# Attention and two feed-forward layers on one core: six spaced batches of transposes a job, a second bank for narrow tiles, layer two's weights kept on chip

## The reference

```python
# q, k, v: (4, 8, 576, 64); token blocks of 64; a row sees its own and earlier blocks
scores = scale * np.matmul(q, k.transpose(0, 1, 3, 2))
scores = np.where(mask, scores, -1000000000.0)
attn = exp(scores - max);  attn = attn / (sum(attn) + 1e-09)
x = (attn @ v) laid out as (2304 tokens, 512)
h = x @ w_in;   x = (h * sigmoid(h)) @ w_out            # d_ff = 2048
h = x @ w_in2;  y = (h * sigmoid(1.702 * h)) @ w_out2
```

## Time and profile before

| | |
|---|---|
| median of 3 runs | 1049.69 us (1048.61 to 1050.72) |
| profiled execution | 1050.25 us, span 1048.5 us |
| PE busy | 991.5 us, 95% |
| DVE, ACT, POOL busy | 44%, 33%, 13% |
| mean granted PE clock | 0.982 |

### The profile page before, as it was taken

The page is one execution under the profiler, slowest core; times in us unless marked ns, Lnnn a source line. Parts: engine busy times, 40 slices in busy tenths (PEclk is TensorE's granted clock), DMA queues, the critical chain, the costliest instruction groups (busy, mean ns, idle before and its releaser), DMA issues.

```text
span 1048.5 us, 13460 instructions
## 1 busy us (share of the span) xinstructions
PE 991.5 (95%) x5256; PEld 778.6 (74%) x5256; DVE 464.5 (44%) x861; ACT 346.4 (33%) x751; POOL 141.3 (13%) x118
## 2 busy tenths in 40 slices
...
GB/s 291 226 252 200 223 231 192 214 202 215 190 213 202 216 192 214 198 213 193 181 185 236 200 198 229 419 198 198 175 231 200 193 201 208 200 185 218 198 312 30
DMA packets 41614, 222.12 MB, mean 212 GB/s; under 512 B 4560, under 2 KB 6096, under 8 KB 19024
## 3 DMA queue, kind: packets, MB, share of 16 engines
...
...
## 4 chain that ended last, share of the span: by engine, by line
PE 78%; DVE 12%; ACT 6%; issue 2%; DMA 2%; POOL 0%; SPq 0%; DVEq 0%; POOLq 0%
PE ps_h L550 12%; PE ps_h L552 12%; PE ps_h L551 12%; PE ps_y L566 11%; PE ps_y L569 10%; PE ps_y L568 10%; PE ps_a L530 4%; DVE p_sb L770 4%; PE ps_a L519 3%; DVE g_f L794 2%; PE ps_a L498 2%; ACT p_sb L637 2%; ACT sig L659 2%; DVE q_lo L752 2%; DMA k_raw<-kT 1%
## 5 line engine op out<-in xcount | busy, mean ns | idle before, releaser
L794 DVE SCALAR_TENSOR_TENSOR g_f<-sig,ps_h 128x512 f32<-128x512 f32 (+1 forms) x160 | 101.3, 633 | 361.1 <-ACT sig L659 361.1
L659 ACT ACTIVATE sig<-ps_h 128x512 f32<-128x512 f32 (+1 forms) x160 | 88.8, 555 | 399.5 <-PE ps_h L552 399.5
L550 PE MATMUL ps_h<-x_hi,w_hl 128*128 128x512 f32 (+1 forms) x444 | 176.3, 397 | 0.3 <-DVE x_lo L746 0.2
L566 PE MATMUL ps_y<-g_hi,w_hl 128*128 128x512 f32 (+1 forms) x444 | 174.6, 393 | 0.5 <-DVE g_lo L800 0.5
L552 PE MATMUL ps_h<-x_lo,w_hl 128*128 128x512 f32 (+1 forms) x444 | 165.8, 373 | 0.0
L569 PE MATMUL ps_y<-g_lo,w_hl 128*128 128x512 f32 (+1 forms) x444 | 165.6, 373 | 0.0
L551 PE MATMUL ps_h<-x_hi,w_hl 128*128 128x512 f32 (+1 forms) x444 | 165.3, 372 | 0.0
L568 PE MATMUL ps_y<-g_hi,w_hl 128*128 128x512 f32 (+1 forms) x444 | 164.7, 371 | 0.0
L800 DVE SCALAR_TENSOR_TENSOR g_lo<-g_f,g_hi 128x512 fp32r<-128x512 f32 (+1 forms) x160 | 105.9, 662 | 72.2 <-ACT g_hi L667 72.2
L667 ACT ACTIVATE g_hi<-g_f 128x512 fp32r<-128x512 f32 (+1 forms) x160 | 94.2, 589 | 109.2 <-DVE g_f L794 108.9
L519 PE MATMUL ps_a<-ident,p_sb 128*128 128x128 f32 x384 | 67.8, 287 | 41.1 <-DVE pt_sb L775 26.4
...
## 6 DMA issues: line engine op xcount, KB each, us to landing
...
```

What stands on the lines that cost most here:

```text
L550: nc.tensor.matmul(dst, lo, x_hi[t % 2][:, k, 0:w], start=(k == 0), stop=False)
L566: nc.tensor.matmul(dst, lo, g_hi[:, c % 2, 0:w], start=(f == 0 and (t > 0 or k % 2 == 0)), stop=False, skip_group_check=True)
L659: nc.scalar.activation(sig[:, 0:w], ps_h[:, 0:w], ACT.Tanh, scale=0.5 * ALPHA[c // SECOND]).then_inc(s_sig, 1)
L794: nc.vector.scalar_tensor_tensor(g_f[:, 0:w], sig[:, 0:w], 1.0, ps_h[:, 0:w], ALU.add, ALU.mult).then_inc(s_g, 1)
```

## The change

1. **Batches.** Eight batches of transposes a job become six of four 128x128 transposes each: the two single ones (row 0's last block, row 7) ride with a batch of three. They are further apart (`BATCH_AT`). ACT and DVE take three batches each; a mixed batch is taken in two copies.
2. **Lanes.** In early jobs the batches alternate between `ps_a`'s bank 2 and `ps_y`'s bank 3, and a batch waits for the take of the batch before the last one. The score rows that had used `ps_y` go back to `ps_a`, so early units wait for the exps of the rows before them (`UNIT_FREE`).
3. **Normalizing.** Row 7 is a group of its own. The places of every DVE and ACT step (`MAX_AFTER` ... `SPLIT_AFTER`) are now tables, for early and later jobs; `queries_low` moves from 14 to 8 places before its job, `keys_low` from 18 to 7 in POOL's order, `keys_high` from 18 to 16.
4. **Two banks.** In 256-token tiles `hidden(c)` alternates between `ps_h` and a spare bank, `g_f` is halved, tanh is written into it in place of `sig`; PE then waits for the gate of chunk `c - 2`. In 512-token tiles one bank remains.
5. **Weights.** `RING` is 6. Layer two's 16 split chunks are loaded once into memory that the attention and layer one used (`w_all`), no longer once a tile.

```diff
-GROUPS = ((0, 1), (1, 3), (3, 5), (5, 8))
+GROUPS = ((0, 1), (1, 3), (3, 5), (5, 7), (7, 8))
...
-BATCHES = [((0,), 0, 4), ((0,), 4, 5), ((1,), 0, 4), ((2,), 0, 4), ((3,), 0, 3), ((4,), 0, 3), ((5, 6), 0, 2), ((7,), 0, 1)]
+BATCHES = ((((0,), 0, 4),), (((1,), 0, 4),), (((2,), 0, 4),), (((3,), 0, 3), ((0,), 4, 5)), (((5, 6), 0, 2),),
+           (((4,), 0, 3), ((7,), 0, 1)))
 NBATCH = len(BATCHES)
-NORMED = (1, 1, 2, 3, 4, 5, 7, 8)
-ON_ACT = {0: 1, 3: 2, 5: 3, 6: 4}
-ON_DVE = {1: 1, 2: 2, 4: 3, 7: 4}
+NORMED = (1, 2, 3, 4, 7, 8)
+ON_ACT = {0: 1, 2: 2, 4: 3}
+ON_DVE = {1: 1, 3: 2, 5: 3}
+N_ON = 3
...
-RING = 4
-MORE = 7
-RING2 = RING + MORE
+RING = 6
+ATT_SLOTS = 8
+STAGE_SLOT = ATT_SLOTS
+RAW_SLOT = ATT_SLOTS + 1
+RING_SLOT = ATT_SLOTS + 2
+SLOT_BYTES = 2 * CW * 4
...
-START = [28 * n - STEP for n in range(FIRST)] + [8 * 13 + 32 * n for n in range(JOBS - FIRST)]
-UNIT_AT = ((0, 5, 10, 15, 20), (0, 6, 12, 18, 24))
-BATCH_AT = ((9, 11, 14, 16, 19, 21, 27, 29), (8, 10, 14, 16, 20, 22, 30, 32))
-PV_AT = (31, 34)
-
-UNIT_FREE = ((0, 0, 1, 3, 5), (0, 1, 3, 5, 7))
+START_AT = (-8, 20, 48, 77, 106)
+START = list(START_AT) + [START_AT[FIRST] + 2 * NF * n for n in range(1, JOBS - FIRST)]
+UNIT_AT = ((0, 5, 9, 13, 21), (0, 6, 14, 18, 26))
+BATCH_AT = ((12, 14, 21, 24, 26, 31), (6, 15, 18, 22, 26, 30))
+PV_AT = (34, 32)
+
+MAX_AFTER = (0, 2)
+EXP_AFTER = ((1, 1), (3, 3))
+INVERT_AFTER = (3, 3)
+MULTIPLY_AFTER = ((6, 6), (4, 5))
+TAKE_AFTER = (-1, 1)
+SPLIT_AFTER = ((1, 2), (1, 2))
+
+PREP_AT = (16, 15, 8, 7)
+
+UNIT_FREE = (0, 1, 3, 5, 7)
...
-PREP = {START[n] - 18: n for n in range(1, JOBS)}
+MAXIMA = {p + MAX_AFTER[late(n)]: (n, u) for p, (n, u) in UNIT.items()}
+EXPS = [{p + EXP_AFTER[late(n)][i]: (n, UNITS[u][i]) for p, (n, u) in UNIT.items() if i < len(UNITS[u])} for i in range(2)]
+INVERT = {p + INVERT_AFTER[late(n)]: (n, u) for p, (n, u) in UNIT.items()}
+MULTIPLY = [{p + MULTIPLY_AFTER[late(n)][i]: (n, u, UNITS[u][i]) for p, (n, u) in UNIT.items() if i < len(UNITS[u])}
+            for i in range(2)]
+TAKE = {p + TAKE_AFTER[late(n)]: (n, b) for p, (n, b) in BATCH.items()}
+SPLIT = [{p + SPLIT_AFTER[late(n)][i]: n for p, n in VALUE.items()} for i in range(2)]
+PREP = [{START[n] - p: n for n in range(1, JOBS)} for p in PREP_AT]
...
+def other(c):
+
+    return c % 2 if TILES[c // NF][1] < TMAX else 0
+
+
+def second_slot(j):
+
+    return j if j < RING_SLOT else RING_SLOT + (j - RING_SLOT + SECOND - RING) % RING
+
+
+def gates_before(c):
+
+    return c - 1 if c and other(c) != other(c - 1) else c
...
-        def row_bank(n, r):
-
-            if n < FIRST and r in (1, 2, 5, 6):
-                return ps_y[:, 512 * (3 - r % 2):512 * (4 - r % 2)]
+        def lane(n, b):
+
+            return ps_y[:, 1536:2048] if n < FIRST and b % 2 else bank(2)
+
+        def row_bank(r):
             return bank(0 if r in (0, 7) else 1 - r % 2)
...
+            if c < SECOND:
+                return w_hl[:, c % RING, low, col:col + P]
+            return w_all[:, second_slot((c - SECOND) % NF), low, col:col + P]
+
+        def hidden_of(c):
+            w = TILES[c // NF][1]
+            spare = ps_y[:, 1024:1024 + w] if c < NF else ps_a[:, 0:w]
+            return spare if other(c) else ps_h[:, 0:w], g_f[:, w * other(c):w * other(c) + w]
...
+            def load_second(j):
+
+                if j == 0:
                     sp.wait_ge(s_xl, NK * PER)
-                else:
-                    sp.wait_ge(s_y, c - RING2 + 1)
-                dst = w_hl[:, s, :, :] if s < RING else w_more[:, s - RING, :, :]
-                sp.dma_start(dst.rearrange("p a c -> p (a c)").bitcast(F32), w_split[i, :, :]).then_inc(s_ld[s], 16)
+                if j == STAGE_SLOT:
+                    sp.wait_ge(s_st, 16 * 2 * NF)
+                if j == RAW_SLOT:
+                    sp.wait_ge(s_w, 2 * NF)
+                if j >= RING_SLOT:
+                    sp.wait_ge(s_y, SECOND - RING + j - RING_SLOT + 1)
+                sp.wait_ge(s_st, 16 * (NF + j + 1))
+                sp.dma_start(w_all[:, second_slot(j), :, :].rearrange("p a c -> p (a c)").bitcast(F32),
+                             w_split[NF + j, :, :]).then_inc(s_l2[j], 16)
...
-                limit = c + 3 if c + 3 < SECOND + RING else c + RING2 - 1
-                while ahead <= min(limit, NCHUNK - 1):
-                    load_split(ahead)
-                    ahead += 1
+                if NF <= c + RING - 1 < SECOND:
+                    load_split(c + RING - 1)
+                if SECOND - NF <= c < SECOND - NF + RING_SLOT:
+                    load_second(c - SECOND + NF)
...
-                    if place in PREP:
-                        keys_low(PREP[place])
+                    if place in PREP[3]:
+                        keys_low(PREP[3][place])
...
-                if n or UNIT_FREE[0][u]:
-                    pe.wait_ge(s_ex, ROWS * n + UNIT_FREE[late(n)][u])
+                if n or u:
+                    pe.wait_ge(s_ex, ROWS * n + UNIT_FREE[u])
...
-                elif b - 1 in ON_ACT:
-                    pe.wait_ge(s_ta, 4 * n + ON_ACT[b - 1])
                 else:
-                    pe.wait_ge(s_td, 4 * n + ON_DVE[b - 1])
+                    before = b - 2 if n < FIRST else b - 1
+                    if before in ON_ACT:
+                        pe.wait_ge(s_ta, N_ON * n + ON_ACT[before])
+                    if before in ON_DVE:
+                        pe.wait_ge(s_td, N_ON * n + ON_DVE[before])
...
+                    if c == 0:
                         pe.wait_ge(s_exl, 2)
+                    elif gates_before(c):
+                        pe.wait_ge(s_g, gates_before(c))
...
+                h, g = hidden_of(c)
+                if gates_before(c):
+                    act.wait_ge(s_gl, gates_before(c))
                 act.wait_ge(s_h, c + 1)
-                nc.scalar.activation(sig[:, 0:w], ps_h[:, 0:w], ACT.Tanh,
-                                     scale=0.5 * ALPHA[c // SECOND]).then_inc(s_sig, 1)
+                nc.scalar.activation(g, h, ACT.Tanh, scale=0.5 * ALPHA[c // SECOND]).then_inc(s_sig, 1)
```

More of the change, by code:

```diff
@@ L166, in build @@
-        k_raw = sb(att, "k_raw", [P, 2, S])
-        q_end = sb(att, "q_end", [P, 2, 2, BLK])
-        q_hi = sb(att, "q_hi", [P, 2, SQ - 2 * BLK], F32R)
-        q_lo = sb(att, "q_lo", [P, 2, SQ - 2 * BLK], F32R)
-        k_hi = sb(att, "k_hi", [P, 2, S], F32R)
-        k_lo = sb(att, "k_lo", [P, 2, S], F32R)
-        v_sb = sb(att, "v_sb", [P, 2, NJ, P])
-        p_sb = sb(att, "p_sb", [P, PCOLS])
-        att.close()
-        w_more = sb(ctx, "w_more", [P, MORE, 2, CW], F32R)
+        first = ExitStack()
@@ new lines, in build @@
+        q_lo = sb(first, "q_lo", [P, 2, SQ - 2 * BLK], F32R)
+        k_hi = sb(first, "k_hi", [P, 2, S], F32R)
+        k_lo = sb(first, "k_lo", [P, 2, S], F32R)
+        v_sb = sb(first, "v_sb", [P, 2, NJ, P])
+        p_sb = sb(first, "p_sb", [P, PCOLS])
+        pt_sb = sb(first, "pt_sb", [P, 2, NJ, SQ])
+        used = 2 * P + 5 * BLK + 4 * ROWS + 2 * (SQ + S) + 4 * (SQ - 2 * BLK + S) + 2 * NJ * P + PCOLS + 2 * NJ * SQ
+        sb(first, "rest", [P, ATT_SLOTS * SLOT_BYTES // 4 - used])
+        stage = sb(first, "stage", [P, 2, CW], F32R)
@@ L223, in build @@
         s_st = sem("s_st")
-        s_ld = [sem(f"s_ld{i}") for i in range(RING2)]
+        s_ld = [sem(f"s_ld{i}") for i in range(RING)]
+        s_l2 = [sem(f"s_l2{i}") for i in range(NF)]
         s_xh = sem("s_xh")
@@ L279, in weights, with pieces @@
-        def weights(c, low, col):
-            s = slot_of(c)
-            ring, s = (w_hl, s) if s < RING else (w_more, s - RING)
-            return ring[:, s, low, col:col + P]
+        def pieces(n, b):
+            col = 0
+            views = []
+            for rows, t0, t1 in BATCHES[b]:
+                w = P * len(rows) * (t1 - t0)
+                flat = lane(n, b)[:, col:col + w]
+                col += w
+                r = rows[0]
+                if r in (0, 7):
+                    dst = pt_sb[:, :, t0:t1, QCOL[r]:QCOL[r] + BLK].rearrange("p h t c -> p t h c")
+                    views.append((dst, flat.rearrange("p (t h c) -> p t h c", h=2, c=BLK)))
+                elif len(rows) == 2:
+                    views.append((pt_sb[:, :, t0:t1, QCOL[r]:QCOL[r] + P],
+                                  flat.rearrange("p (h t c) -> p h t c", h=2, c=P)))
+                else:
+                    views.append((pt_sb[:, (r + 1) % 2, t0:t1, QCOL[r]:QCOL[r] + P],
+                                  flat.rearrange("p (t c) -> p t c", c=P)))
+            return views
@@ L352, in _ @@
             y_out = out.rearrange("(k p) t -> p k t", p=P)
-            ahead = NF
             for c in range(-1, NCHUNK):
@@ L641, in take_batch @@
                 act.wait_ge(s_tr, NBATCH * n + b + 1)
-                dst, src = batch_views(b)
-                nc.scalar.activation(dst, src, ACT.Copy).then_inc(s_ta, 1)
+                for dst, src in pieces(n, b):
```

(2 more changed lines are left out.)

205 lines of the change are left out of this document (87 added, 118 removed).

## The result

The changed kernel takes **997.3 us** (median of four runs, 994.6 to 999.3) against 1049.2 us for the one before in the same session: a ratio of 0.950, 95% interval 0.947 to 0.953. I had forecast 1019 us, range 1005 to 1035. The profiled execution took 999.31 us with a span of 997.5 us, 51.0 us less than before.

A forecast was written before the change was run, and what follows sets the result against it. PE, busy 95% of the span, bounds the kernel through idle time and clock. First tile -6.7 (waits) and -6.0 (clock), later jobs -16.4 and -1.5 (clock), make -30.6 us: 1050.25 - 30.6 - 0.56 gives 1019 us, range 1005 to 1035.

The forecast's parts named there:

- First tile: Layer one's first tile, early jobs: PE's waits -6.7 us, 12 of 18.7 us staying, and clock -6 us.
- the clock: First tile: PE's four half-clock stretches partly go with smaller waits, -6 us, bounds 0 and -9.
- The 1.0 us a job at the next unit 0: First tile: PE waits 1.0 us at the next job's unit 0, whose exp stands behind `q_lo`.
- rival A: First tile: DVE is the bound, so new waits replace those for copies and nothing is gained there; 1032 us, chance 0.15.
- Later jobs, what stays: Twelve later jobs: 6.0 of 22.4 us of PE's waits stay, 2.4 at row 7 and 3.6 from splits; bounds 2 and 18.
- Later jobs, -16.4: Twelve later jobs: `q_lo` behind the copy and four places between batches cut PE's waits by 16.4 us.
- Merging single transposes: 0: Every job: no gain, as transposes stay 24 and copies 8 a job; extra small DVE instructions run beside PE's work.
- Weights on chip: 0: Layer two: loads fall from 80 to 16 but PE waited for none and kept its pitch; priced 0 to +1 us.
- Two banks: 0: Narrow tiles: a second bank gains 0 by itself, since no wait of PE is for a gate; bounds 0 and -1.
- Ring of 6: First tile: POOL may run two chunks further ahead, so SP issues job 4's keys sooner; counted in the first tile.
- Rival B: Nearly all waits go: the burst falls in slack, 6 us stay, no half-clock stretch; 1004 us, chance 0.17.
- C: Later jobs: values wait for the last batch's copies, 12 x 3.7 = 44 us lost; 1057 us, chance 0.05.

The follow-up runs named there:

- experiment 1: The changed kernel run again, unedited, as base for the other experiments: 997.5 us (five runs), ratio 0.951 to the kernel before.
- experiment 9: The changed kernel with the splits of keys and queries at their old places (18, 16, 14 and 18 before the job): 1000.1 us, ratio 0.953.
- experiment 5: The changed kernel with later jobs' second and fourth batches moved to one place ahead of their successors: 1004.9 us, ratio 0.957.
- experiment 4: The changed kernel with each batch of four transposes in the twelve later jobs cut into two halves, one step apart: 1007.1 us, ratio 0.960.
- experiments 2 and 3: Kernel before, 128 unused bytes ahead of `x_hi1`: 1042.5 us; changed kernel, 64, 128 or 256 bytes between `g_lo` and the weights: 1010.1, 1010.4, 999.9 us.
- experiment 2: The kernel before with 128 bytes a partition of unused memory ahead of `x_hi1`, all loads still there: 1042.5 us, ratio 0.994.
- experiment 6: The changed kernel with one bank for the first product of 256-token tiles: 997.0 us, ratio 0.950.
- experiment 8: The changed kernel with POOL held four chunks behind in place of six, the ring keeping its six slots: 1000.2 us, ratio 0.953.

## Why the prediction was right and wrong

**First tile: right in its mechanism, near in its sum partly by luck.** Forecast 12.7 us, measured 14.2 in the profiled execution and 4 more in another. Two terms missed in opposite directions. The waits of these 16 chunks fell by 9.4 us (20.1 to 10.7) and not by 6.7, the clock gave 3 us and not 6, and some 2 us of PE's own time stand in no term. The 1.0 us a job at the next unit 0 is 0.3 us once. The wait before unit (3, 4) of job 0 was to be 1.6 us, and those at the fifth batch 1.4 us each:

```profile
27.15 0.44 PE L530 MATMUL ps_a<-k_hi,q_lo 64*128 64x384 f32 x2 [1.70 <-ACT p_sb L686]
...
41.08 0.66 PE L566 MATMUL ps_a<-ident,p_sb 128*128 128x128 f32 x4 [2.28 <-DVE p_sb L817]
```

The other two are 1.41 and 1.80 us. The cause is the burst of POOL, as the prediction had it. DVE, then POOL:

```profile
37.20 1.00 DVE L810 TENSOR_SCALAR den_e<-den 128x2 f32<-128x2 f32 x1
38.24 0.17 DVE L812 RECIPROCAL rden<-den_e 128x2 f32<-128x2 f32 x1
38.44 2.58 DVE L817 TENSOR_SCALAR p_sb<-p_sb,rden 128x256 f32<-128x256 f32 x2
```

```profile
37.01 1.17 POOL L452 CAST w_hl<-w_raw 128x1024 fp32r<-128x1024 f32 x1
38.26 2.61 POOL L455 TENSOR_TENSOR w_hl<-w_raw,w_hl 128x512 fp32r<-128x512 f32 x2
```

Two multiplications take 2.58 us beside POOL; alone, in a later job, 0.61 (next rows). These have one input in SBUF, so of the rule the prediction weighed it is the part on two-port modes that bears on them (the Trainium skill, SBUF — State Buffer, "Who interferes with whom": whoever issues first holds the shared pair for its whole instruction); the trace agrees, 1.29 us each beside 1.3 us of POOL. The rule did not make DVE the bound (rival A): PE lost 10.9 us of 93. The clock gave less: PE is busy 12.3 us in the half-clock stretches in place of 18.0, which costs 6.1 us in place of 9.0, so -3 and not -6. As the stretches vary between executions (6.8 us in all in experiment 1, 13.6 here), this term was never known to better than some 3 us.

**Later jobs, what stays: too much.** Forecast 6.0 us, measured 1.5 (2.2 in experiment 1). DVE in a later job after:

```profile
198.53 0.17 DVE L810 TENSOR_SCALAR den_e<-den 128x2 f32<-128x2 f32 x1 [0.22 <-ACT p_sb L686]
198.74 0.17 DVE L812 RECIPROCAL rden<-den_e 128x2 f32<-128x2 f32 x1
198.94 0.61 DVE L817 TENSOR_SCALAR p_sb<-p_sb,rden 128x256 f32<-128x256 f32 x2
199.68 0.76 DVE L822 COPY pt_sb<-ps_a 128x384 f32<-128x384 f32 x2
200.35 0.55 DVE L799 SCALAR_TENSOR_TENSOR q_lo<-q_raw,q_hi 128x384 fp32r<-128x384 f32 x1
```

`q_lo` follows the copy and takes 0.55 us, not the 1.64 us of the earlier trace rows, since `k_lo` no longer runs beside it. The steady 0.2 us a job that I had put before the last batch do not exist: the last multiplications end before PE asks. Of the meetings with POOL I had counted four at 0.9 us; PE waits three times, for copies, 0.3 to 0.8 us each. Of the two reasons that the prediction gave, the four places between batches alone do nearly all: with `q_lo` and `k_lo` at their old places chunks 16 to 64 take 381.4 us (experiment 9), with two of the distances drawn together and the new places 386.5 (experiment 5). What the move of `q_lo` would give at the old distances no run shows.

**Later jobs, what goes: too little.** A wait before transposes costs more than its row says. The kernel before:

```profile
215.75 0.39 PE L568 MATMUL ps_y<-g_hi,w_hl 128*128 128x512 f32 x1
215.98 0.40 PE L569 MATMUL ps_y<-g_lo,w_hl 128*128 128x512 f32 x1
217.22 0.52 PE L519 MATMUL ps_a<-ident,p_sb 128*128 128x128 f32 x3 [0.85 <-DVE pt_sb L775]
217.50 0.47 PE L566 MATMUL ps_y<-g_hi,w_hl 128*128 128x512 f32 x1
217.81 0.39 PE L568 MATMUL ps_y<-g_hi,w_hl 128*128 128x512 f32 x1
218.04 0.40 PE L569 MATMUL ps_y<-g_lo,w_hl 128*128 128x512 f32 x1
```

From 215.98 to 217.22 is 1.24 us. Less 0.85 of waiting, 0.39 is left for a matmul whose pitch is 0.23: the listed wait begins only where the profile has the last matmul end (its ends are modelled). So this wait cost 1.24 - 0.23 = 1.01 us, not 0.85. Over the later jobs the last matmul ahead of a waiting batch takes 0.39 us 25 times, and 0.235 ahead of one that does not wait: 3.9 us that no row calls idle. The first matmul behind a batch takes 0.31 to 0.32 us (217.50 to 217.81) in place of 0.23. There were 148 first matmuls behind a batch, a unit or values in the steps, now 93: 5.0 us less; against it stand transposes in wider batches, which take 2.7 us more. A last term of 1.1 us are matmuls ahead of units and values, 67 and now 57 at 0.32 us.

The later jobs' 29.5 us are then 19.4 of listed waits (forecast 16.4, out of 20.9 in these chunks), 3.9 of draining, 3.4 of interruptions, about 2 of clock (forecast 1.5) and, left over, about 1. Two steps of the prediction failed here. The first is "*Later jobs, -16.4*": it took a wait to be worth what its row says, where 25 of them cost 0.16 us more each (3.9 us), and it let 6.0 us stay where 1.5 do. The second is "*Merging single transposes: 0*" with its reason that the number of transposes stays: the steps are interrupted less often, 3.4 us by this count. That count is taken from two traces that differ in much else, and no run isolates it. Experiment 4 puts a lower price on it: with 72 more interruptions and 12 more waits that drain, PE's own time grew by 2.9 us, 1.9 of it for the 12. An interruption alone is thus dear by 0.01 us there and by 0.06 here; what is dear is a wait.

**Weights on chip: 0, and wrong by 6.2 us for a reason that has nothing to do with loads.** This step failed too, and experiments 2 and 3 show what stood in its place: the placement of the operands. The prediction read layer two's pitch at 600 to 700 us, but 44 of those 100 us lie ahead of chunk 80 (644.4 us), in layer one's last tile, where all operands start at the same offset. At 1010 and 1030 us it compared traffic rightly, but in a tile of 256 tokens, where offsets cost nothing. Between them, from 660 to 940 us, the row above would have shown 4.34 matmuls a us in place of 4.40. That loads cost PE nothing is confirmed by experiment 2; that "moved into layer one's memory" also changes the offsets of every operand was not thought of. The prediction's own sign for this, fewer than 440 matmuls in 100 us, could not show it, since the error was a gain.

**Two banks: 0, right** (experiment 6). **Ring of 6: the reason was wrong.** The keys of job 4 are now issued at 91.70 us, not at 103.36, and ACT splits them without waiting. But they are issued at 90.14 us with POOL held four chunks behind too (experiment 8), so it is not the ring that brings them forward. Its worth is at most some 4 us.

**The sum.** 51.0 us of span against 30.6: layer two 6.2, later jobs 11.6, first tile 1.5, prologue 1.2, which is the 20.4 that were missing. The profiled execution lay 2.0 us above its median, and the forecast had put in 0.6, another 1.4; 1019.1 - 20.4 - 1.4 = 997.3. The prediction's "own range" of 1009 to 1029 does not follow from its bounds either: half of them is 8.5 us down and 16 up, 1011 to 1035. Rival B came nearest in its time (1004), but not by its mechanism: 12.4 us of waits and three half-clock stretches stay, where it had 6 and none. C did not happen: values wait for nothing. Of the signs, waits for `p_sb` are gone from the later jobs; one wait of 0.82 us for a copy stays there (1.10 in experiment 1), where none of 0.85 was to be; and the clock has three low stretches, not one or two.
